# The check of w on GpSimd and its flag on ScalarE, in a fused attention and two-layer kernel

## Chip, core and metric

The kernel runs on one core of one Trainium2 chip. The metric is the device time of one execution in microseconds; smaller is better. The program before took 919.12 us, the median of three runs (918.99 to 919.40).

## What is computed

The reference is a linear attention with a decaying state, followed by two feed-forward layers, all in float32:

```python
for t in range(S):                       # S = 768, B = 4, H = 8, D = 48
    cur = einsum('bhd,bhe->bhde', u * k[t], v[t])
    y[t] = einsum('bhd,bhde->bhe', r[t], state + cur)
    state = w * state + einsum('bhd,bhe->bhde', k[t], v[t])
x = y.transpose(0, 2, 1, 3).reshape(B * S, H * D)      # 3072 x 384
x = ((x @ w_a) * (x @ w_b)) @ w_out                    # d_ff 1536
h = x @ w_in;  g = h * clip(h + 3, 0, 6) / 6
out = g @ w_out2                                       # d_ff 2048
```

w holds one decay for each of the 8 x 48 places, drawn between 0.85 and 0.95.

## The kernel before

The attention is computed by chunks of 128 steps: 6 chunks of the sequence times 4 batches are 24 chunks. Within a chunk r and k are scaled by powers of w and by their inverses, so that the decay becomes a product of matrices; masks take the part above the diagonal away, and the weight of a step on itself, from u, is put on the diagonal. Such powers only stay in range when w does. So the program first looks whether all of w lies in 0.75 to 1.33 (`W_MIN`, `W_MAX`). It makes a flag, every engine reads the flag (`decide`) and branches: to the chunked form, or to a general path that steps through the sequence. With these inputs the chunked form is taken.

The feed-forward layers split each float32 operand into a high and a low part and add three products. TensorE does the first four chunks ahead of layer 1; the 20 others are woven into layer 1 at fixed slots, then layer 2 follows. The engines run their own instruction streams, written out by hand, and meet at semaphores.

The change lies in the first microseconds, before the branch. There the order is this:

- **SyncE** (`first_loads`) issues the load of w and u (`w_u_col`), then `first_rk` for four chunks and `first_v` for two, then reads the flag and goes on with the weights (`w_raw`).
- **GpSimd** fills `three` and builds the masks (`make_masks`: one memset and eight selects, L487), clears the state (L1270), and reads the flag.
- **VectorE** (`guard_and_tables`) clears `zeros` (L1192) and sets the ones of the power table (L1193). It waits for w, compares it with both bounds (L1196 and L1198, results in `in_range`), scans the powers of w (L1201, four scans), takes TensorE's count, compares it (L1204) and turns it into an integer flag (L1206). Then come two reciprocals (L1208, L1209), the product r times k of the first chunk (L1049, waits for the first `first_rk`), the second table (L591), and its own reading of the flag. In `vector_fast` follow the scaling of r and k (L1044) and the masks (L1067, L1072).
- **ScalarE** makes a first activation, so that its table is loaded (L1279), and reads the flag. Then it copies the scale of the keys (L994), later the own weights of the first chunk (L1002), and from them eight diagonals (L854).
- **TensorE** multiplies zeros, to be kept busy (`keep_warm`, L756; the number is that of 128 columns), counts what is in range by four matmuls of one column (L1293), multiplies zeros again, then computes the own weights of the first chunk (L630) and its weights (L614) in `first_chunks`.

The tests for the count are a sum of 3.0 over 112 partitions x 4 columns: 1344 when all is in range.

Of the kernel before, what the change touches and what calls it, by code (L numbers as in the profile page):

```python
# [20 lines left out]
ALU = mybir.AluOpType  # L21
ACT = mybir.ActivationFunctionType
AX = mybir.AxisListType

P = 128
# [13 lines left out]
W_MIN, W_MAX = 0.75, 1.33  # L39
# [8 lines left out]
def build(nc, r, k, v, w, u, w_a, w_b, w_out, w_in2, w_out2, rk_turned, natural, w_u_pairs, outT):  # L48
# [11 lines left out]
    NP = H // 2  # L60
# [18 lines left out]
    with ExitStack() as ctx:  # L79
# [27 lines left out]
        with ExitStack() as setup:  # L107

            in_range = sb("in_range", [P, NP], of=setup)
            all_in = sb("all_in", [1, 1], of=setup)  # L110
            inv_fine = sb("inv_fine", [P, NP, FINE + 1], of=setup)
            inv_coarse = sb("inv_coarse", [P, NP, COARSE + 1], of=setup)
            zeros = sb("zeros", [P, CH], of=setup)
            tab_sT = sb("tab_sT", [P, NP, CH], of=setup)
# [192 lines left out]

        count_ps = acc_ps[0:1, 1, 0:1]
        HD = H * D
# [166 lines left out]


        def make_masks(pool):

# [16 lines left out]
            keep_where(P, every, 1, -1, MID, 1, ALU.is_equal)  # L496
            keep_where(P + MID, every, 1, -1, 0, 1, ALU.is_equal)
            keep_where(2 * P, low_half, 1, -1, 0, 1, ALU.is_gt)
            keep_where(late, every, 1, -1, MID, NP // 2, ALU.is_gt)
# [683 lines left out]

        def guard_and_tables(dve):

            links = [0]

            def link(ins):
# [6 lines left out]
            dve.wait_ge(s_w_u, 16)  # L1195
            dve.tensor_scalar(in_range[0:W2], w_col[0:W2], W_MIN, None, ALU.is_ge).then_inc(s_guard, 1)  # L1196
            dve.wait_ge(s_guard, 1)
            dve.scalar_tensor_tensor(out=in_range[0:W2], in0=w_col[0:W2], scalar=W_MAX, in1=in_range[0:W2],  # L1198
                                     op0=ALU.is_le, op1=ALU.mult).then_inc(s_guard, 1)
            for p in range(NP):  # L1200
                link(dve.tensor_tensor_scan(power[0:W2, p, 1:CH + 1], w_col[0:W2, p:p + 1].to_broadcast([W2, CH]),  # L1201
                                            zeros[0:W2, :], 1.0, ALU.mult, ALU.add))
            dve.wait_ge(s_count, 1)
            dve.tensor_scalar(all_in[:], count_ps, 3.0 * W2 * NP - 1.0, None, ALU.is_ge).then_inc(s_guard, 1)  # L1204
            dve.wait_ge(s_guard, 3)
            dve.tensor_copy(flag[:], all_in[:]).then_inc(s_flag, 1)  # L1206
            dve.wait_ge(s_set, links[0])
# [47 lines left out]
        with nc.Block() as block:  # L1255
# [10 lines left out]
            @block.gpsimd  # L1266
            def _(pool):
                nc.gpsimd.memset(three[:], 3.0).then_inc(s_three, 1)
                make_masks(pool)
                nc.gpsimd.memset(state[:], 0.0).then_inc(s_zero, 1)  # L1270
                flag_pool = decide(pool)
                with pool.If(flag_pool == 1):
                    pool_fast(pool)
                with pool.Else():
                    pool_general(pool)
            @block.scalar
            def _(act):
                act.wait_ge(s_three, 1)
                nc.scalar.activation(first_use[:], three[:], ACT.Copy)  # L1279
                flag_act = decide(act)  # L1280
                with act.If(flag_act == 1):
                    scalar_fast(act)
                with act.Else():
                    scalar_general(act)
                evacuate_last(act)
            @block.tensor
            def _(pe):
                pe.wait_ge(s_set, 1)
                keep_warm(pe, 4)
                pe.wait_ge(s_three, 1)  # L1290
                pe.wait_ge(s_guard, 2)
                for p in range(NP):
                    mm = pe.matmul(count_ps, in_range[0:W2, p:p + 1], three[0:W2, :], start=(p == 0), stop=(p == NP - 1))  # L1293
                mm.then_inc(s_count, 1)
                keep_warm(pe, 4)
                keep_warm(pe, 2)
                first_chunks(pe)
# [3 lines left out]
            def _(dve):  # L1301
                guard_and_tables(dve)
                flag_dve = decide(dve)
# [176 lines left out]
```

## Time and profile before

| | |
|---|---|
| median of three runs | 919.12 us (918.99 to 919.40) |
| the profiled execution's own time | 919.12 us |
| its span, first to last instruction | 917.3 us |
| TensorE busy | 911.9 us (99%) |
| VectorE busy | 369.5 us (40%) |
| ScalarE busy | 329.5 us (36%) |
| GpSimd busy | 184.3 us (20%) |

The profile is of one execution. The own time is longer than the span by what lies before the first and behind the last instruction. PE is TensorE, PEld its weight loads, DVE VectorE, ACT ScalarE, POOL GpSimd, and SPq the queue of SyncE that issues DMAs. A duration of a timeline row that merges several instructions (x4) reaches from the start of the first to the end of the last. The chain is followed back from the last instruction, at each step to what released it.

### The profile page before, as it was taken

The numbers are of one execution on the slowest core, as the hardware profiler recorded it, in microseconds if no ns is written. First come the engines' busy times: TensorE is split into PE (matmuls) and PEld (weight loads), VectorE is DVE, ScalarE is ACT, GpSimd is POOL, SyncE is SP. The second block draws the span as 40 slices with busy tenths as digits, with TensorE's granted clock in tenths as the row PEclk, the third lists the DMA queues.
The fourth block names the chain that finished last, engine by engine and source line by source line (L and its number), as shares of the span: only waits on it lengthen the run. The fifth ranks groups of instructions, "written<-read, shape, count | busy, mean of one in ns | idle before, by whom it ended". The sixth has DMA issues, their size and how long they took to land.

```text
span 917.3 us, 15108 instructions
## 1 busy us (share of the span) xinstructions
PE 911.9 (99%) x6400; PEld 746.4 (81%) x6400; DVE 369.5 (40%) x607; ACT 329.5 (36%) x651; POOL 184.3 (20%) x168
## 2 busy tenths in 40 slices
PE   8999999999999999999999999999999999999998
PEld 6788888888888888888888888888888888888887
DVE  7746344525443343334222343343343343343332
ACT  6645323232333233242221343433333333333333
POOL 5976102111111111010755570000000000000000
PEclk9999999999999999999999999999999999999999
DMA  8653211121120121131311210100200100100000
GB/s 307 198 167 108 90 50 62 55 90 56 56 110 34 56 110 55 38 129 48 115 50 55 78 50 1 65 5 1 69 1 0 70 1 7 64 0 1 35 1 36
DMA packets 24281, 57.84 MB, mean 63 GB/s; under 512 B 2320, under 2 KB 8080, under 8 KB 24208
## 3 DMA queue, kind: packets, MB, share of 16 engines
q1 hardware_dynamic: 19808, 48.18, 15.6%
q10 hardware_dynamic: 4400, 8.65, 2.5%
q8 instruction: 50, 0.82, 0.4%
q14 instruction: 23, 0.19, 0.1%
HBM read 47.39 MB, written 9.44 MB: 62 GB/s over the span
## 4 chain that ended last, share of the span: by engine, by line
PE 98%; DVE 1%; DMA 0%; ACT 0%; issue 0%; SPq 0%; DVEq 0%; ACTq 0%
PE up_ps L722 32%; PE up_ps L799 21%; PE acc_ps L736 16%; PE acc_ps L813 11%; PE att_ps L813 11%; PE att_ps L614 2%; PE att_ps L677 1%; PE att_ps L682 1%; PE att_ps L646 1%; PE att_ps L663 1%; PE att_ps L671 1%; DMA first_rk<-in_rk_turned 0%; ACT A L854 0%; DVE first_rk L1044 0%; DVE first_A L1067 0%
## 5 line engine op out<-in xcount | busy, mean ns | idle before, releaser
L722 PE MATMUL up_ps<-x_cut,w_up 128*128 128x512 f32 x1296 | 307.3, 391 | 0.2 <-ACT x_cut L867 0.2
L722 PEld LDWEIGHTS up_ps<-x_cut,w_up 128*128 128x128 f32 x1296 | 241.7, 188 | 52.9 <-issue 3.0
L926 ACT ACTIVATE g_cut<-tmp 128x512 fp32r<-128x512 f32 x168 | 106.2, 632 | 214.4 <-DVE tmp L1149 141.6
L1157 DVE SCALAR_TENSOR_TENSOR g_cut<-tmp,g_cut 128x512 fp32r<-128x512 f32 x168 | 125.2, 745 | 117.5 <-ACT g_cut L926 117.5
L736 PE MATMUL acc_ps<-g_cut,w_down 128*128 128x512 f32 x648 | 157.3, 390 | 0.0
L736 PEld LDWEIGHTS acc_ps<-g_cut,w_down 128*128 128x128 f32 x648 | 121.3, 188 | 26.0 <-issue 0.6
L1151 DVE SCALAR_TENSOR_TENSOR tmp<-tmp,up_ps 128x512 f32<-128x512 f32 x96 | 66.1, 689 | 182.9 <-ACT tmp L920 182.9
L920 ACT ACTIVATE tmp<-up_ps,three 128x512 f32<-128x512 f32 x96 | 66.2, 690 | 171.0 <-PE up_ps L799 171.0
L1149 DVE TENSOR_TENSOR tmp<-tmp,up_ps 128x512 f32<-128x512 f32 x72 | 49.5, 688 | 169.7 <-PE up_ps L722 169.6
L799 PE MATMUL up_ps<-x_cut,w_up 128*128 128x512 f32 x432 | 105.7, 389 | 0.0
L799 PE MATMUL up_ps<-x_cut,w_in_first 128*128 128x512 f32 x432 | 105.4, 389 | 0.0
L799 PEld LDWEIGHTS up_ps<-x_cut,w_up 128*128 128x128 f32 x432 | 81.1, 188 | 16.8
L799 PEld LDWEIGHTS up_ps<-x_cut,w_in_first 128*128 128x128 f32 x432 | 81.1, 188 | 16.8
L918 ACT ACTIVATE tmp<-up_ps 128x512 f32<-128x512 f32 x72 | 43.0, 598 | 112.4 <-PE up_ps L722 112.4
L513 POOL TENSOR_TENSOR nat<-nat 128x384 f32<-128x384 f32 x20 | 23.6, 1180 | 278.9 <-DMA nat<-in_natural 278.9
L813 PE MATMUL att_ps<-g_cut,w_up 128*128 128x512 f32 x324 | 79.3, 389 | 0.0
L813 PE MATMUL acc_ps<-g_cut,w_up 128*128 128x512 f32 x324 | 79.3, 389 | 0.0
L813 PEld LDWEIGHTS att_ps<-g_cut,w_up 128*128 128x128 f32 x324 | 60.8, 188 | 12.6
L813 PEld LDWEIGHTS acc_ps<-g_cut,w_up 128*128 128x128 f32 x324 | 60.8, 188 | 12.6
L854 ACT ACTIVATE A<-masks_sb,own 128x128 f32<-128x128 f32 x160 | 50.3, 388 | 5.6 <-DVE own L1060 5.6
L243 POOL TENSOR_TENSOR w_up<-w_raw,w_up 128x512 fp32r<-128x512 f32 (+2 forms) x42 | 47.3, 1140 | 6.9 <-ACT w_up L237 5.2
L1101 DVE TENSOR_TENSOR x_cut<-att_ps,x_cut 128x384 fp32r<-128x384 f32 x21 | 11.7, 557 | 60.3 <-ACT x_cut L867 60.3
(109 smaller groups left out, 557.2 us busy)
## 6 DMA issues: line engine op xcount, KB each, us to landing
nat<-in_natural SPq DMA_DIRECT2D x20, 704.0 KB, 6.0
rkT<-in_rk_turned SPq DMA_DIRECT2D x20, 512.0 KB, 3.6
w_raw<-in_moe_w_out SPq DMA_DIRECT2D x28, 192.0 KB, 2.4
layer_out_T<-stage ACTq DMA_DIRECT2D x6, 768.0 KB, 3.4
x_cut<-layer_out_T SPq DMA_DIRECT2D x6, 768.0 KB, 4.3
outT<-stage ACTq DMA_DIRECT2D x5, 768.0 KB, 3.3
w_raw<-in_moe_w_in SPq DMA_DIRECT2D x12, 256.0 KB, 4.6
first_rk<-in_rk_turned SPq DMA_DIRECT2D x4, 512.0 KB, 5.6
```

Source lines behind the costliest of these rows:

```text
L243: nc.gpsimd.tensor_tensor(out=pieces[m][1](LO), in0=raw_of(m), in1=pieces[m][1](HI).bitcast(F32), op=ALU.subtract).then_inc(s_w_cut, 1)
L722: mm = pe.matmul(up_ps[:, m, :], w_up[i // PB][:, a, m, c, cols], x_cut[:, t % 2, b, c, :], start=(z == 0), stop=(z == len(order) - 1))
L736: mm = pe.matmul(acc_ps[:, j, :], w_down[:, a, i, j * P:(j + 1) * P], g_cut[:, (t * N1 + i) % GR, b, :], start=(i == 0 and z == 0), stop=( ...
L799: mm = pe.matmul(up_ps[:, i % 2, :], in2_at(a, c, i), x_cut[:, t % 2, b, c, :], start=(c == 0 and z == 0), stop=(c == KC - 1 and z == 2))
L813: mm = pe.matmul(sums(t)[:, j, :], wo2_at(a, i)[:, j * P:(j + 1) * P], g_cut[:, n % GR, b, :], start=(i == 0 and z == 0), stop=(last and z ...
L854: ins = nc.scalar.activation(A_at(q, half)[:, p, :], id_sb[p // 2], ACT.Copy, scale=mine[:, h:h + 1])
L918: nc.scalar.activation(tmp[:, i % 2, :], src, ACT.Copy).then_inc(s_act1, 1)
L920: nc.scalar.activation(tmp[:, i % 2, :], src, ACT.Relu, bias=three[:, 0:1]).then_inc(s_act1, 1)
L926: nc.scalar.activation(g_cut[:, n % GR, HI, :], tmp[:, n % 2, :], ACT.Copy, scale=1.0 if n < TILES * N1 else 1.0 / 6.0).then_inc(s_gh, 1)
L1149: dve.tensor_tensor(out=tm, in0=tm, in1=up_ps[:, 1, :], op=ALU.mult).then_inc(s_g, 1)
L1151: dve.scalar_tensor_tensor(out=tm, in0=tm, scalar=6.0, in1=up_ps[:, n % 2, :], op0=ALU.min, op1=ALU.mult).then_inc(s_g, 1)
L1157: dve.scalar_tensor_tensor(out=lo, in0=tmp[:, n % 2, :], scalar=1.0 if n < TILES * N1 else 1.0 / 6.0, in1=hi.bitcast(F32), op0=ALU.mult, o ...
```

## The change

Both comparisons of w go from VectorE to GpSimd (`find_in_range`): two comparisons into two tiles and a product of the two, between the fourth and the fifth select of `make_masks`. The flag is now made by ScalarE, in one activation that reads TensorE's count in PSUM: Relu(count + 1 - 1344) is 1 when all is in range and 0 otherwise, and is written as an integer. The bias stands in a tile of one value, `all_but_one`, that GpSimd fills first. TensorE's wait for the comparisons goes from the second to the third step of their semaphore, the count lies in another bank of PSUM (`att_ps` in place of `acc_ps`), and the last of the two warming matmuls behind the count has 128 columns instead of 256. `guard_and_tables` becomes `tables_of_powers`. The order of SyncE's loads stays.

```diff
--- before.py
+++ after.py
@@ -107,7 +107,8 @@
         with ExitStack() as setup:
 
             in_range = sb("in_range", [P, NP], of=setup)
-            all_in = sb("all_in", [1, 1], of=setup)
+            not_above = sb("not_above", [P, NP], of=setup)
+            all_but_one = sb("all_but_one", [1, 1], of=setup)
             inv_fine = sb("inv_fine", [P, NP, FINE + 1], of=setup)
             inv_coarse = sb("inv_coarse", [P, NP, COARSE + 1], of=setup)
             zeros = sb("zeros", [P, CH], of=setup)
@@ -305,7 +306,7 @@
         def x_view(tile, z, q):
             return x_cut[:, tile % 2, z, :, cols_of(q)]
 
-        count_ps = acc_ps[0:1, 1, 0:1]
+        count_ps = att_ps[0:1, 0, 0:1]
         HD = H * D
         by_head = lambda x: x.rearrange("s (h d) -> s h d", h=H)
         A_of = lambda q: first_A[:, q % 2] if 2 <= q < B else A[:, q % 2]
@@ -475,6 +476,15 @@
                 sp.dma_start(outT_v[:, j, cols], st[:, j, :]).then_inc(s_st, 16)
 
 
+        def find_in_range(pool):
+
+            pool.wait_ge(s_w_u, 16)
+            nc.gpsimd.tensor_scalar(in_range[0:W2], w_col[0:W2], W_MIN, None, ALU.is_ge).then_inc(s_guard, 1)
+            nc.gpsimd.tensor_scalar(not_above[0:W2], w_col[0:W2], W_MAX, None, ALU.is_le).then_inc(s_guard, 1)
+            pool.wait_ge(s_guard, 2)
+            nc.gpsimd.tensor_tensor(out=in_range[0:W2], in0=in_range[0:W2], in1=not_above[0:W2],
+                                    op=ALU.mult).then_inc(s_guard, 1)
+
         def make_masks(pool):
 
 
@@ -495,6 +505,7 @@
             keep_where(MID, every, 1, -1, MID, 1, ALU.is_equal)
             keep_where(P, every, 1, -1, MID, 1, ALU.is_equal)
             keep_where(P + MID, every, 1, -1, 0, 1, ALU.is_equal)
+            find_in_range(pool)
             keep_where(2 * P, low_half, 1, -1, 0, 1, ALU.is_gt)
             keep_where(late, every, 1, -1, MID, NP // 2, ALU.is_gt)
             keep_where(late + NP // 2 * MID, low_half, 1, -1, 0, NP // 2, ALU.is_gt)
@@ -1181,7 +1192,7 @@
                     if i == 4 and t + 1 < TILES:
                         x2_low(dve, t + 1)
 
-        def guard_and_tables(dve):
+        def tables_of_powers(dve):
 
             links = [0]
 
@@ -1193,17 +1204,9 @@
             link(dve.memset(power[:, :, 0:1], 1.0))
             dve.wait_ge(s_set, links[0])
             dve.wait_ge(s_w_u, 16)
-            dve.tensor_scalar(in_range[0:W2], w_col[0:W2], W_MIN, None, ALU.is_ge).then_inc(s_guard, 1)
-            dve.wait_ge(s_guard, 1)
-            dve.scalar_tensor_tensor(out=in_range[0:W2], in0=w_col[0:W2], scalar=W_MAX, in1=in_range[0:W2],
-                                     op0=ALU.is_le, op1=ALU.mult).then_inc(s_guard, 1)
             for p in range(NP):
                 link(dve.tensor_tensor_scan(power[0:W2, p, 1:CH + 1], w_col[0:W2, p:p + 1].to_broadcast([W2, CH]),
                                             zeros[0:W2, :], 1.0, ALU.mult, ALU.add))
-            dve.wait_ge(s_count, 1)
-            dve.tensor_scalar(all_in[:], count_ps, 3.0 * W2 * NP - 1.0, None, ALU.is_ge).then_inc(s_guard, 1)
-            dve.wait_ge(s_guard, 3)
-            dve.tensor_copy(flag[:], all_in[:]).then_inc(s_flag, 1)
             dve.wait_ge(s_set, links[0])
             link(dve.reciprocal(inv_fine[0:W2], fine[0:W2]))
             link(dve.reciprocal(inv_coarse[0:W2], coarse[0:W2]))
@@ -1266,6 +1269,7 @@
             @block.gpsimd
             def _(pool):
                 nc.gpsimd.memset(three[:], 3.0).then_inc(s_three, 1)
+                nc.gpsimd.memset(all_but_one[:], 1.0 - 3.0 * W2 * NP).then_inc(s_three, 1)
                 make_masks(pool)
                 nc.gpsimd.memset(state[:], 0.0).then_inc(s_zero, 1)
                 flag_pool = decide(pool)
@@ -1275,8 +1279,11 @@
                     pool_general(pool)
             @block.scalar
             def _(act):
-                act.wait_ge(s_three, 1)
+                act.wait_ge(s_three, 2)
                 nc.scalar.activation(first_use[:], three[:], ACT.Copy)
+
+                act.wait_ge(s_count, 1)
+                nc.scalar.activation(flag[:], count_ps, ACT.Relu, bias=all_but_one[:, 0:1]).then_inc(s_flag, 1)
                 flag_act = decide(act)
                 with act.If(flag_act == 1):
                     scalar_fast(act)
@@ -1288,18 +1295,18 @@
                 pe.wait_ge(s_set, 1)
                 keep_warm(pe, 4)
                 pe.wait_ge(s_three, 1)
-                pe.wait_ge(s_guard, 2)
+                pe.wait_ge(s_guard, 3)
                 for p in range(NP):
                     mm = pe.matmul(count_ps, in_range[0:W2, p:p + 1], three[0:W2, :], start=(p == 0), stop=(p == NP - 1))
                 mm.then_inc(s_count, 1)
                 keep_warm(pe, 4)
-                keep_warm(pe, 2)
+                keep_warm(pe, 1)
                 first_chunks(pe)
                 tensor_layer1(pe)
                 tensor_layer2(pe)
             @block.vector
             def _(dve):
-                guard_and_tables(dve)
+                tables_of_powers(dve)
                 flag_dve = decide(dve)
                 with dve.If(flag_dve == 1):
                     vector_fast(dve)
```

VectorE, from the memset of the power table to the reciprocals. Names in brackets are the semaphores waited for: `w_and_u_loaded` is the load of w and u, `in_range_counted` TensorE's count. Before:

```order
L1193 MEMSET tab_rk 128x4
L1196 TENSOR_SCALAR in_range<-w_u_col 112x4 [waits w_and_u_loaded,table_chain]
L1198 SCALAR_TENSOR_TENSOR in_range<-w_u_col,in_range 112x4 [waits guard_chain]
L1201 SCALAR_TENSOR_TENSOR tab_rk<-w_u_col,zeros 112x128 x4
L1204 TENSOR_SCALAR all_in<-acc_ps 1x1 [waits in_range_counted]
L1206 CAST flag<-all_in 1x1 [waits guard_chain]
L1208 RECIPROCAL inv_fine<-tab_rk 112x68 [waits table_chain]
L1209 RECIPROCAL inv_coarse<-tab_rk 112x36
L1049 TENSOR_TENSOR prod<-first_rk 112x512 [waits first_rk_loaded0]
```

The same place in the changed program:

```order
L1204 MEMSET tab_rk 128x4
L1208 SCALAR_TENSOR_TENSOR tab_rk<-w_u_col,zeros 112x128 [waits w_and_u_loaded,table_chain]
L1208 SCALAR_TENSOR_TENSOR tab_rk<-w_u_col,zeros 112x128 x3
L1211 RECIPROCAL inv_fine<-tab_rk 112x68 [waits table_chain]
L1212 RECIPROCAL inv_coarse<-tab_rk 112x36
L1060 TENSOR_TENSOR prod<-first_rk 112x512 [waits first_rk_loaded0]
```

Four instructions are gone, and with them the wait for TensorE's count; the scans wait for the load of w themselves.

GpSimd, from its first memset to the memset of the state, before:

```order
L1268 MEMSET three 128x1
L492 MEMSET masks_sb 128x576
L487 ISA
L487 AFFINE_SELECT masks_sb<-masks_sb 128x64 [waits ones_set]
L487 AFFINE_SELECT masks_sb<-masks_sb 128x64 x3
L487 AFFINE_SELECT masks_sb<-masks_sb 64x64
L487 AFFINE_SELECT masks_sb<-masks_sb 128x128
L487 AFFINE_SELECT masks_sb<-masks_sb 64x128
L487 AFFINE_SELECT masks_sb<-masks_sb 64x64 [waits masks_made]
L1270 MEMSET state_fast 128x1024 [waits masks_made]
```

And in the changed program, from the second memset to the last select:

```order
L1272 MEMSET all_but_one 1x1
L502 MEMSET masks_sb 128x576
L497 ISA
L497 AFFINE_SELECT masks_sb<-masks_sb 128x64 [waits ones_set]
L497 AFFINE_SELECT masks_sb<-masks_sb 128x64 x3
L482 TENSOR_SCALAR in_range<-w_u_col 112x4 [waits w_and_u_loaded]
L483 TENSOR_SCALAR not_above<-w_u_col 112x4
L485 TENSOR_TENSOR in_range<-in_range,not_above 112x4 [waits guard_chain]
L497 AFFINE_SELECT masks_sb<-masks_sb 64x64
L497 AFFINE_SELECT masks_sb<-masks_sb 128x128
L497 AFFINE_SELECT masks_sb<-masks_sb 64x128
L497 AFFINE_SELECT masks_sb<-masks_sb 64x64 [waits masks_made]
```

One memset and three instructions on w have come in, the latter with a wait for the load in front of the last four selects.

ScalarE, from its start to the first work behind the branch, in the changed program (before, the row with `flag<-att_ps,all_but_one` is missing, and nothing else differs):

```order
L1283 ACT_TABLE_LOAD
L1283 ACTIVATE first_use<-three 128x1 [waits three_set]
L1286 ACTIVATE flag<-att_ps,all_but_one 1x1 [waits in_range_counted]
L1256 TENSOR_LOAD flag [waits flag_ready]
L1256 ISA x2
L1288 COMPARE_AND_BRANCH
L1005 ACTIVATE tab_sT<-tab_rk 112x256 [waits table_chain]
```

The new row waits for TensorE's count, and ScalarE's own reading of the flag stands behind it.

## Rows read from the trace of the kernel before

**Rows 1.** The page: span, and busy time of each engine.

```profile
span 917.3 us, 15108 instructions
...
PE 911.9 (99%) x6400; PEld 746.4 (81%) x6400; DVE 369.5 (40%) x607; ACT 329.5 (36%) x651; POOL 184.3 (20%) x168
```

**Rows 2.** The page: shares of the chain that ended last.

```profile
PE 98%; DVE 1%; DMA 0%; ACT 0%; issue 0%; SPq 0%; DVEq 0%; ACTq 0%
```

**Rows 3.** The chain in order of time: start us, duration us, what.

```profile
1.25 3.95 DMA first_rk<-in_rk_turned
...
5.23 0.70 DVE prod L1049
...
5.97 1.06 PE acc_ps L630 x12
...
7.13 0.18 ACT own_first L1002
...
7.34 2.45 ACT A L854 x8
...
9.91 0.74 DVE A L1067
...
20.55 2.37 PE up_ps L722 x9
```

**Rows 4.** Timeline of VectorE, 0 to 8 us: start, us, engine, line, what.

```profile
2.60 0.17 DVE L1196 TENSOR_SCALAR in_range<-w_u_col 112x4 f32<-112x4 f32 x1 [1.52 <-DMA w_u_col<-in_w_u_pairs]
2.80 0.17 DVE L1198 SCALAR_TENSOR_TENSOR in_range<-w_u_col,in_range 112x4 f32<-112x4 f32 x1
2.89 1.36 DVE L1201 TENSOR_TENSOR_SCAN tab_rk<-w_u_col,zeros 112x128 f32<-112x128 f32 x4
4.17 0.12 DVE L1204 TENSOR_SCALAR all_in<-acc_ps 1x1 f32<-1x1 f32 x1
4.33 0.14 DVE L1206 CAST flag<-all_in 1x1 int32<-1x1 f32 x1
4.40 0.56 DVE L1208 RECIPROCAL inv_fine<-tab_rk 112x68 f32<-112x68 f32 x1
4.88 0.31 DVE L1209 RECIPROCAL inv_coarse<-tab_rk 112x36 f32<-112x36 f32 x1
```

**Rows 5.** Timeline of GpSimd, before and at the scans: same columns.

```profile
0.80 0.10 POOL L1268 MEMSET three<- 128x1 f32 x1 [0.29 <-POOLq L1433]
...
1.48 0.24 POOL L487 TENSOR_SCALAR_AFFINE_SELECT masks_sb<-masks_sb 128x64 f32<-128x64 f32 x1
...
3.02 0.32 POOL L487 TENSOR_SCALAR_AFFINE_SELECT masks_sb<-masks_sb 64x64 f32<-64x64 f32 x1
...
3.40 0.95 POOL L1270 MEMSET state_fast<- 128x1024 f32 x1
```

**Rows 6.** TensorE's timeline; then one stretch, granted clock third number from the end.

```profile
3.12 0.34 PE L1293 MATMUL acc_ps<-three,in_range 112*1 112x1 f32 x8
...
3.39 2.02 PE L756 MATMUL up_ps<-zeros 128*128 128x512 f32 x2
...
4.41 1.22 PE L756 MATMUL up_ps<-zeros 128*128 128x512 f32 x2
...
5.25 0.59 PE L756 MATMUL up_ps<-zeros 128*128 128x256 f32 x2
...
6.95 1.12 PE L756 MATMUL up_ps<-zeros 128*128 128x512 f32 x2
...
1.00:2.00 1.00, 0.88 (x1) 0.50 (x2) 0.08 (x2) 1.00 (x1) 0.93 (x4) 1.00 0.05 3
```

**Rows 7.** Timeline of SyncE's queue and of ScalarE.

```profile
3.14 1.18 SPq L366 DMA_DIRECT2D first_v<-in_natural  x2
...
5.34 0.82 ACT L994 ACTIVATE tab_sT<-tab_rk 112x256 f32<-112x256 f32 x3 [3.04 <-DVE inv_coarse L1209]
5.40 0.94 SPq L232 DMA_DIRECT2D w_raw<-in_moe_w_a  x2
```

## The prediction

> **What bounds the kernel now.** The page comes first, for the span and the engines' busy time. The span is 917.3 us and TensorE is busy in 911.9 of it [rows 1], so only 5.4 us of its time are not matmuls. The shares of the chain that ended last say the same: 98% is PE, and DVE has 1% [rows 2]. A change to four VectorE instructions of 0.1 to 0.2 us can therefore only tell where TensorE isn't yet the bound, which is the start. For that I read the chain in order of time, and its first pieces are the argument [rows 3]. It begins with the load of the first `first_rk`, which lands at 1.25 + 3.95 = 5.20 us. Behind it come VectorE's product (5.23), TensorE's own products (5.97), ScalarE's copy and eight diagonals (7.13 to 9.79) and VectorE's first mask (9.91). About ten more microseconds of such hand-overs lead to 20.55 us, where layer 1 begins on TensorE, and from there the chain is TensorE nearly throughout. The change edits only what lies between 0.8 and 5.9 us. So the question is whether the product at 5.23 or the matmuls at 5.97 can start at another time.
>
> The product sits on a near tie. VectorE's timeline [rows 4] has the second reciprocal at 4.88 for 0.31 us, so VectorE is free at 5.19; the load lands at 5.20. VectorE is as late as the load, but no later.
>
> **The change on VectorE.** It loses the two comparisons (L1196 and L1198) and the two instructions of the flag (L1204 and L1206). The scans now start when w lands, at 2.60 where the first comparison stood, instead of at 2.89 [rows 4]: 0.29 us earlier, so they end at 2.60 + 1.36 = 3.96. The reciprocals follow their last result directly. They started at 4.40 behind the flag; from the first start to the end of the second they take 5.19 - 4.40 = 0.79, so they now end at about 3.98 + 0.79 = 4.77. VectorE is ready for the product 0.42 us earlier. The product still waits for the load at 5.20, and SyncE's queue ahead of that load is unchanged (w and u first, then the four `first_rk`). The gain on the path is 5.19 to 5.20, so **nothing**; the 0.42 us become a wait for DMA. This is where the gain stops. The bounds are 0 and 0.42 us, and I take 0.
>
> **On GpSimd.** A memset of one value is added; the one in front of it, `three`, took 0.10 [rows 5], so at most 0.10. Then three instructions on 112x4 stand between the fourth select and the fifth. The trace has no such instruction on this engine. Its nearest rows are a memset of one column per partition, 0.10, and selects on 128x64 and 64x64, 0.24 and 0.32 [rows 5]. I take 0.20 each, near the select, since it too reads and writes, with fewer elements here. Four selects from 1.58 on, of 0.24 at most, are done by 2.54, so the wait for w (2.60) is what starts the three. The first two overlap to 0.3 in all, the third waits for both and takes 0.20, and with 0.05 for the hand-over that is 2.60 + 0.55 = 3.15; by the upper bound, 3 x 0.32 = 0.96, it is 3.56. The four later selects, the memset of the state and GpSimd's reading of the flag move back by 0.5 to 1.0 us. Before, the selects ended at 3.34 and the state's memset at 4.35 [rows 5], and their first readers are ScalarE at 7.13 [rows 3] and later, so a microsecond is covered twice over.
>
> The Trainium skill, GPSIMD Engine Reference, section Engine selection, speaks against this move: two-input elementwise work is about twice as slow there as on VectorE. With twice the 0.17 us of L1196 for each of the three, an estimate by that page, the end is 2.60 + 1.02 = 3.62, within 0.1 of my upper bound, and the sum stays the same.
>
> **On TensorE.** The count (four matmuls of one column, 0.34 us) started at 3.12, when the first warming matmul let it [rows 6]. It now waits for GpSimd: 3.20, or 3.65 by the upper bound; call the lateness d, 0.1 to 0.5 us. Behind it stand the warming matmuls, first 512 columns, then 256, which the change cuts to 128. What follows them matters: the own products at 5.97, which waited for VectorE's product, not for TensorE, free at 5.25 + 0.59 = 5.84. From the starts [rows 6]: one pass of 512 columns took 4.41 - 3.39 = 1.02 us, the next 5.25 - 4.41 = 0.84, and at 6.95 two took 1.12, or 0.56 each. The granted clock reads 1.00 already in the stretch from 1 to 2 us, which is the upper level, 2.4 GHz, and TensorE works there 0.88 of the time. But the passes nearly halve, so I read that the array really rose from the lower level, 1.2 GHz, after it had been busy from about 1.1 us on, and with 0.84 between 1.02 and 0.56, at 4.41 + 0.61 x 1.02 = 5.03. After the change with d = 0.1: the second pass starts at 4.51, does 0.51 of itself until 5.03 and the rest by 5.30; two passes of 128 columns at a quarter of 0.56 end at 5.58. With d = 0.5 the end is 5.80. TensorE meets 5.97 as long as d is below about 0.75, that is, GpSimd done by 3.85. Cost: nothing; the cover is TensorE's idle time before 5.97.
>
> **On ScalarE and SyncE.** The flag is made by one activation of 1x1 from PSUM: 0.18 us by the copy of 128x8 from PSUM [rows 3], 0.10 after the count ends, as between the end of the own products at 5.97 + 1.06 = 7.03 and 7.13. So the flag is ready at 3.20 + 0.34 + 0.10 + 0.18 = 3.82 (4.3 by the upper bound) instead of 4.33 + 0.14 = 4.47. ScalarE sat idle for the 3.04 us before 5.34 [rows 7], so nothing is queued behind its new wait except its own reading of the flag. SyncE can't use all of this: its issue of `first_v` runs from 3.14 to 4.32 [rows 7], and before it waited only from there to the flag at 4.47. Its first w_raw issue moves from 5.40 to about 5.25, and the issues behind it too. These transfers queue behind those that the chain needs, on the same queue, and no piece of the chain before 20.55 waits for one; worth 0. VectorE reads the flag after it has dispatched the product and the table, as before.
>
> **Sum.** Product 0, own products 0, flag 0: 0.0 us on the profiled execution. Its own time is 919.12 us, equal to the median of the three runs (919.12), so I predict 919.1. A measurement of this kernel can tell about 0.2% (1.8 us) from no change, and all the time on the path between 2.60 and 5.97 is 3.4 us.
>
> **Rivals.** *GpSimd is held by VectorE's scans, and TensorE is late.* Both now start when w lands, both read it, and the scans run back to back until 3.96. If GpSimd's instructions wait for all four, they end at 3.96 + 0.60 = 4.56 and the count at 4.60 + 0.34 = 4.94; that is d = 1.5, past the deciding 0.75. With the clock risen at 5.03 as before, 2.5 passes end at 5.03 + (2.5 - 0.09) x 0.56 = 6.38: 0.4 us late, 919.5. If the idle 1.4 us put off the rise of the clock as well, they end at 4.94 + 2.5 x 1.02 = 7.49 (+1.5), and the own products, 1.06 long, may double (+1.1). Then ScalarE's copy and diagonals, and with them the mask at 9.91, come 2.6 us late: 921.7, slower. Against it speaks the last select: it ran from 3.02 to 3.34 [rows 5], wholly beside the scans that began at 2.89 [rows 4], and took 0.32 where it should have been held to the end of a scan first. For it: 0.32 is more than 0.24. I give the mild form 0.07 and the hard one 0.05.
>
> The Trainium skill, SBUF — State Buffer, section Who interferes with whom, has this as a rule: a VectorE instruction with two SBUF inputs holds off a GpSimd instruction that reads SBUF, for its whole length. By that rule the mild form or worse should come; the trace's select of 0.32 agrees at most in part.
>
> *The load is not the last to arrive.* In the profiled execution load and VectorE are 0.01 us apart. If in most executions the load lands earlier than 5.20, the chain gains what VectorE gave up, up to 0.42 us: 918.7. For it speaks the tie alone, which would be a coincidence; against it, that the trace names the load and that the times of three runs lie within 0.4 us. Chance 0.13.
>
> *The change doesn't do what it says:* an activation with Relu could bring a second table load in front of the flag. The built program has one load on ScalarE in both kernels, and ScalarE's 3 us of idle time would take much of another. It changes no time and I fold it into the forecast.
>
> **How the numbers follow.** Forecast (within 0.3 us of 919.1) 0.71; a gain by the early load, 0.13, 918.7; GpSimd held with the clock in time, 0.07, 919.5; with the clock late, 0.05, 921.7; anything else, 0.04, half of it faster by over 0.2% and half within. The slower case is 2.6 us, over the 1.8 us; all other listed ones are below it. So faster 0.02, same 0.71 + 0.13 + 0.07 + 0.02 = 0.93, slower 0.05. The range reaches from the early load, less 0.2 for the spread of the runs, 918.5, to the mild form of the first rival, plus 0.3 for the same, 919.8. It leaves out the hard form.
>
> **What would show it.** In the profile after: VectorE's scans start at 2.6 and its reciprocals end near 4.8, followed by a new wait of about 0.4 us for `first_rk`; GpSimd's three instructions end between 3.1 and 3.6; the count starts just behind; flag at 3.8 to 4.3; product at 5.2, own products near 5.97, first mask at 9.9, layer 1 at 20.5. I'm wrong if the own products start after 6.1 (TensorE late), if the second warming pass no longer shortens (clock), or if the product starts clearly before 5.2 (the load was not the bound).

## The result and the profile after

| | before | changed |
|---|---|---|
| median | 919.50 us, 22 runs | 924.02 us, 22 runs |
| lowest to highest | 918.94 to 920.11 | 918.88 to 925.07 |
| profiled execution | 919.12, span 917.3 | 924.59, span 922.9 |

The ratio is 1.0034, with a 95% interval of 1.0023 to 1.0045: slower, and outside the forecast range of 918.5 to 919.8. It follows the means, here and below; the medians alone give 1.0049. In the runs below, three executions far outside all others, which no run explains, are left out of counts, medians and ratios: one of 3280 us with the kernel before, one of 1534 in e2 and one of 1533 in e8. The median tells less than the single times. Of the 22 executions 6 took 918.9 to 919.9 us, as before; 4 took 920.9 to 921.8; 12 took 924.0 to 925.1. The kernel before has its 22 within 1.2 us. The change has made the time fall into three groups.

The page of the changed kernel, whose profiled execution is of the slowest group:

```profile
span 922.9 us, 15107 instructions
...
PE 917.5 (99%) x6400; PEld 751.6 (81%) x6400; DVE 368.8 (40%) x603; ACT 329.4 (36%) x652; POOL 185.3 (20%) x172
...
PE 99%; ACT 0%; DMA 0%; DVE 0%; issue 0%; POOL 0%; DVEq 0%
```

Against [rows 1] TensorE is busy for 5.6 us more with as many matmuls, and against [rows 2] VectorE's 1% has left the chain. The chain in order of time says where (start, duration, what):

```profile
0.80 1.59 DMA w_u_col<-in_w_u_pairs
...
3.09 0.21 POOL in_range L485
3.30 0.14 issue
3.44 0.34 PE att_ps L1300 x8
3.77 2.43 PE up_ps L767 x4
6.21 1.37 PE acc_ps L641 x12
7.58 2.01 PE up_ps L767 x2
9.58 1.49 PE up_ps L625 x32
11.07 1.67 PE acc_ps L641 x12
...
20.97 0.18 ACT own_first L1013
...
25.93 2.34 PE up_ps L733 x9
```

Layer 1 begins at 25.93 instead of 20.55 [rows 3], 5.38 of the span's 5.6 us. The other 0.2 is not placed. From 3.44 to 20.94 the chain is TensorE without a break, where before it was a relay of four engines.

The timelines of VectorE, GpSimd and ScalarE, each in its first microseconds:

```profile
2.49 1.43 DVE L1208 TENSOR_TENSOR_SCAN tab_rk<-w_u_col,zeros 112x128 f32<-112x128 f32 x4 [1.41 <-DMA w_u_col<-in_w_u_pairs]
3.96 0.58 DVE L1211 RECIPROCAL inv_fine<-tab_rk 112x68 f32<-112x68 f32 x1
4.45 0.32 DVE L1212 RECIPROCAL inv_coarse<-tab_rk 112x36 f32<-112x36 f32 x1
5.03 0.69 DVE L1060 TENSOR_TENSOR prod<-first_rk 112x512 f32<-112x512 f32 x1 [0.26 <-DMA first_rk<-in_rk_turned]
```

```profile
2.46 0.24 POOL L482 TENSOR_SCALAR in_range<-w_u_col 112x4 f32<-112x4 f32 x1
2.78 0.22 POOL L483 TENSOR_SCALAR not_above<-w_u_col 112x4 f32<-112x4 f32 x1
3.09 0.20 POOL L485 TENSOR_TENSOR in_range<-in_range,not_above 112x4 f32<-112x4 f32 x1
```

```profile
3.81 0.25 ACT L1286 ACTIVATE flag<-att_ps,all_but_one 1x1 int32<-1x1 f32 x1 [1.52 <-PE att_ps L1300]
```

These came nearly as forecast. VectorE is free at 4.77 (forecast 4.77), waits 0.26 us for the load, and the product starts 0.20 us earlier than before, since here the load landed at 5.0. GpSimd ends at 3.29 (forecast 3.15 to 3.56), the flag at 4.06 (3.8 to 4.3). What is different is TensorE's timeline:

```profile
1.12 2.07 PE L767 MATMUL up_ps<-zeros 128*128 128x512 f32 x2 [1.12 <-DVE tab_rk L1204]
3.44 0.34 PE L1300 MATMUL att_ps<-three,in_range 112*1 112x1 f32 x8 [0.24 <-POOL in_range L485]
3.70 2.50 PE L767 MATMUL up_ps<-zeros 128*128 128x512 f32 x4
6.00 1.58 PE L641 MATMUL acc_ps<-w_u_col,prod 112*128 112x64 f32 x12
7.51 2.08 PE L767 MATMUL up_ps<-zeros 128*128 128x512 f32 x2
...
15.18 1.58 PE L641 MATMUL acc_ps<-w_u_col,prod 112*128 112x64 f32 x12
...
18.55 1.40 PE L625 MATMUL up_ps<-first_rk 48*64 48x128 f32 x32
19.89 1.04 PE L641 MATMUL acc_ps<-w_u_col,prod 112*128 112x64 f32 x12
```

The own products of the first chunk start at 6.00, as before (5.97), but the warming pair of 512 columns behind them takes 2.08 us where it took 1.12 [rows 6]. The next own products take up to 1.7 us until 16.8 and 1.04 only at 19.89. Only TensorE is slower: ScalarE's copy `own_first` takes 0.18 us and VectorE's product 0.69 in both kernels. I read from these durations that TensorE ran at the lower of its two levels, 1.2 GHz, until about 19.7 us, within the row at 18.55; before, it rose to 2.4 GHz ahead of 5.97. The granted clock does not show it. The table of stretches gives it as the third number from the end, and in this stretch, with slow passes throughout, it reads 1.00, the upper level:

```profile
8.00:9.00 1.00, 1.00 (x2) 0.01 (x1) 0.90 (x2) 1.00 (x4) 0.00 (x0) 1.00 1.00 384
```

### The profile page after: what moved, and what is told of

It reads as the page before. It is cut to its first block, busy times and chain, and to the rows that moved or that the text cites. A ratio compares the mean times of both kernels' runs of the same rounds, so it can differ in the third digit from the quotient of the medians.

```text
span 922.9 us, 15107 instructions
## 1 busy us (share of the span) xinstructions
PE 917.5 (99%) x6400; PEld 751.6 (81%) x6400; DVE 368.8 (40%) x603; ACT 329.4 (36%) x652; POOL 185.3 (20%) x172
## 4 chain that ended last, share of the span: by engine, by line
PE 99%; ACT 0%; DMA 0%; DVE 0%; issue 0%; POOL 0%; DVEq 0%
PE up_ps L733 32%; PE up_ps L810 21%; PE acc_ps L747 16%; PE acc_ps L824 11%; PE att_ps L824 11%; PE att_ps L625 2%; PE att_ps L688 1%; PE att_ps L693 1%; PE att_ps L657 1%; PE att_ps L674 1%; PE acc_ps L641 1%; PE att_ps L682 1%; PE up_ps L767 0%; PE up_ps L625 0%; PE acc_ps L688 0%; DMA w_u_col<-in_w_u_pairs 0%
## 5 line engine op out<-in xcount | busy, mean ns | idle before, releaser
L810 PEld LDWEIGHTS up_ps<-x_cut,w_in_first 128*128 128x128 f32 x432 | 81.1, 188 | 16.8
L810 PEld LDWEIGHTS up_ps<-x_cut,w_up 128*128 128x128 f32 x432 | 81.1, 188 | 16.8
```

What stands on the lines that cost most here:

```text
L810: mm = pe.matmul(up_ps[:, i % 2, :], in2_at(a, c, i), x_cut[:, t % 2, b, c, :], start=(c == 0 and z == 0), stop=(c == KC - 1 and z == 2))
```

## The experiments

The question is which part of the change puts off the rise of the clock. Three things changed ahead of 6 us on TensorE: it waits 0.24 us for GpSimd ahead of the count (the gap), it does 128 warming columns less, and the count comes at 3.44 instead of 3.12. Below, 512 | 512, 256 means the warming columns ahead of the count and behind it. Executions are sorted by time into "early" (under 920.4 us), "middle" (to 923.6) and "late" (up to 925.7); the names are those of the rise of the clock, which the profiles place at 5.3 to 8, at about 11, and at about 20 us. The gap is that of the one profiled execution.

| kernel | warming | gap in the profile | early | middle | late | median |
|---|---|---|---|---|---|---|
| before, 125 executions | 512 \| 512, 256 | none | 123 | 2 | 0 | 919.3 to 919.8 |
| changed | 512 \| 512, 128 | 0.24 | 6 | 4 | 12 | 924.02 |
| e1 | 512 \| 512, 256 | 0.28 | 4 | 3 | 5 | 922.61 |
| e2 (of before) | 512 \| 512, 128 | 0.13 | 2 | 5 | 3 | 921.74 |
| e3 | 512, 128 \| 512 | none | 5 | 4 | 3 | 921.04 |
| e4 | 512 \| 512, 512 | 0.49 | 1 | 6 | 4 | 921.07 |
| e5 | 512 \| 512, 256 | none | 11 | 0 | 0 | 919.61 |
| e6 | 512 \| 512, 256 | 0.28 | 5 | 2 | 3 | 920.84 |
| e7 | 512, 128 \| 512, 128 | none | 8 | 2 | 1 | 920.00 |
| e8 | 512, 256 \| 384 | none | 6 | 1 | 4 | 919.47 |
| e9 (of before) | 512 \| 512, 256 | 0.29 | 5 | 2 | 5 | 922.09 |
| e10 and e11 | 512, 256 \| 512 | none | 20 | 2 | 0 | 919.12, 919.17 |

The cuts of the code below are shown against the changed kernel for e1, e3, e4, e7, e8, e10 and e11, and against the kernel before for e2, e5, e6 and e9; `...` stands for lines left out.

### e1: the 256 columns restored

```diff
                 keep_warm(pe, 4)
-                keep_warm(pe, 1)
+                keep_warm(pe, 2)
```

> The changed kernel, with the second warming matmul behind the count at 256 columns, as before, instead of 128. In the changed kernel's profile TensorE's passes of 512 columns still take 1.04 us at 7.51 (0.56 before), and everything on it up to about 19 us is slow: that is the loss. Theory A (the gap): what puts off the rise is that TensorE waits for GpSimd from 3.19 to 3.44 us. The gap is untouched here, so the times stay spread between 919 and 925 with a median over 922. Theory B (the shorter warming): what puts it off is the 128 columns taken away. Then the times fall back to 919.0 to 920.0, median 919.4, or less by the 0.2 us by which the load landed earlier.

Measured: 922.61 us, 919.79 to 924.99; ratio 1.0033, 1.0020 to 1.0046. As theory A expected. A third is early: with the gap the rise is uncertain even with all columns. Its profiled execution (924.83):

```profile
3.47 0.34 PE L1300 MATMUL att_ps<-three,in_range 112*1 112x1 f32 x8 [0.28 <-POOL in_range L485]
3.74 2.93 PE L767 MATMUL up_ps<-zeros 128*128 128x512 f32 x4
...
5.61 1.06 PE L767 MATMUL up_ps<-zeros 128*128 128x256 f32 x2
...
6.46 1.58 PE L641 MATMUL acc_ps<-w_u_col,prod 112*128 112x64 f32 x12
7.97 2.08 PE L767 MATMUL up_ps<-zeros 128*128 128x512 f32 x2
```

The same four passes took 2.45 us before (3.39 to 5.84) and take 2.93 here, and the own products start 0.5 us later for it. (The row at 5.61 is the last two of the four, from a narrower stretch of the timeline.)

### e2: the shorter warming alone

```diff
                 keep_warm(pe, 4)
-                keep_warm(pe, 2)
+                keep_warm(pe, 1)
```

> The kernel before, with that warming matmul cut to 128 columns and nothing else: no gap before the count, which starts at 3.12. Theory A: 919.0 to 920.1 as before, and passes of 0.56 us at 6.95. Theory B: spread from 919 to 925, median over 921.

Measured: 921.74 us (921.93 with the execution of 1534 us), ratio 1.0030, 1.0017 to 1.0043. This is theory B's outcome, where e1 was A's. Neither alone is right: each part by itself puts off the rise. (In the profiled execution w landed late enough for a gap of 0.13 us as well.) The profiled execution (922.12) is of the middle group and shows what sets it apart, a rise at about 11 us:

```profile
6.04 1.74 PE L630 MATMUL acc_ps<-w_u_col,prod 112*128 112x64 f32 x12
...
9.72 1.56 PE L614 MATMUL up_ps<-first_rk 48*64 48x128 f32 x32
11.21 1.04 PE L630 MATMUL acc_ps<-w_u_col,prod 112*128 112x64 f32 x12
```

### e3: the 128 columns ahead of the count

```diff
                 keep_warm(pe, 4)
+                keep_warm(pe, 1)
                 pe.wait_ge(s_three, 1)
...
                 keep_warm(pe, 4)
-                keep_warm(pe, 1)
```

> The changed kernel, with the 128 columns moved from behind the count to ahead of it, so that TensorE still works while GpSimd compares; behind the count stand 512 columns alone. The sum of columns is the changed kernel's. Theory A: the gap of 0.25 us closes to under 0.1 and the times go back to 919.0 to 920.0. Theory B (too few columns): as the changed kernel, 919 to 925, median over 922; or worse, since TensorE then idles before its own products at about 5.8.

Measured: 921.04 us, 918.74 to 924.72; ratio 1.0019, 1.0004 to 1.0034. Neither theory's numbers: 5 of 12 are early, against 6 of 22 for the changed kernel, too few to call it better. With the gap closed the lack of columns is left.

### e4: 512 columns in the last warming matmul

```diff
-                keep_warm(pe, 1)
+                keep_warm(pe, 4)
```

> The changed kernel, with the second warming matmul at 512 columns instead of 128. TensorE is then busy until about 7.4 us by slow passes, or 6.5 if the clock rises in them, and the own products (ready at 5.7) start later than 6.0. Theory A: the rise still depends on the gap, so the spread stays and each time is up to 1.5 us longer, median over 923. Theory B: the rise always comes, and the cost is what the own products wait: 919.5 to 920.5, median near 920.

Measured: 921.07 us, 920.36 to 925.70; ratio 1.0030, 1.0016 to 1.0044. Neither theory fits. Seven of 11 lie at 920.4 to 921.1 and four at 925.4 to 925.7. I take the seven for early rises that pay for the own products' lateness; the one profile is of a late execution (925.53), so that isn't shown. More columns behind the gap may help (7 of 11 against 6 of 22), and don't make up for it. In the profile w came later too, and the gap was 0.49.

### e5: the flag on ScalarE alone

```diff
-            dve.wait_ge(s_count, 1)
-            dve.tensor_scalar(all_in[:], count_ps, 3.0 * W2 * NP - 1.0, None, ALU.is_ge).then_inc(s_guard, 1)
-            dve.wait_ge(s_guard, 3)
-            dve.tensor_copy(flag[:], all_in[:]).then_inc(s_flag, 1)
...
+                act.wait_ge(s_count, 1)
+                nc.scalar.activation(flag[:], count_ps, ACT.Relu, bias=all_but_one[:, 0:1]).then_inc(s_flag, 1)
```

> One part of the change alone: VectorE compares as before, ScalarE makes the flag, the warming matmuls as before (512 | count | 512, 256). The count starts near 3.1 us again, with no gap ahead of it. Theory A2 (the rise of the clock comes early only when TensorE is busy almost without a break from 1.1 to 6 us; a gap of 0.25 us ahead of the count or 0.3 us more behind the last warming pass each spoil it): no break, so 919.0 to 920.1, median 919.4. Rival D (what spoils it is the flag's new place, through the transfers and reads behind it that come earlier): spread from 919 to 925, median over 921.

Measured: 919.61 us, 919.03 to 919.92; ratio 1.0003, 0.9994 to 1.0012. All 11 early, as theory A2 expected. Nothing that the flag's new place costs or brings is clear of the noise. The profile:

```profile
3.17 0.34 PE L1303 MATMUL att_ps<-three,in_range 112*1 112x1 f32 x8
3.44 2.93 PE L766 MATMUL up_ps<-zeros 128*128 128x512 f32 x4
6.16 1.12 PE L640 MATMUL acc_ps<-w_u_col,prod 112*128 112x64 f32 x12
7.21 1.12 PE L766 MATMUL up_ps<-zeros 128*128 128x512 f32 x2
```

Here the clock rose at about 6.3, behind the warming passes instead of within them, and the own products are already near 1.04. They start 0.2 us later, and the execution took 919.57. So a rise a microsecond later than before still counts as early.

### e6: the comparisons on GpSimd alone

```diff
-            dve.tensor_scalar(in_range[0:W2], w_col[0:W2], W_MIN, None, ALU.is_ge).then_inc(s_guard, 1)
...
+            find_in_range(pool)
...
-                pe.wait_ge(s_guard, 2)
+                pe.wait_ge(s_guard, 3)
```

> The other part alone: GpSimd compares, VectorE makes the flag as before, the warming matmuls as before. The gap of 0.25 us ahead of the count is there. Theory A2: spread like the changed kernel with 256 columns restored (919.8 to 925, median 922.6). Rival D: 919.0 to 920.1.

Measured: 920.84 us, 919.25 to 925.40; ratio 1.0027, 1.0011 to 1.0043. The spread is there, five of ten executions above 920.4. So the loss comes with the comparisons, not with the flag. The profiled execution (919.91) is an early one, with the gap of 0.28 that stood before a late rise in e1:

```profile
6.46 1.35 PE L642 MATMUL acc_ps<-w_u_col,prod 112*128 112x64 f32 x12
7.75 1.13 PE L768 MATMUL up_ps<-zeros 128*128 128x512 f32 x2
```

The clock rose at about 7.3, within the own products. The size of the gap alone doesn't decide when.

### e7 and e8: warming that covers the wait for GpSimd

```diff
                 keep_warm(pe, 4)
+                keep_warm(pe, 1)
                 pe.wait_ge(s_three, 1)
```

> The changed kernel with 128 columns more, ahead of the count: 512, 128 | count | 512, 128. The sum of columns is that of the kernel before and of the run with 256 restored, which had a median of 922.6; only the gap ahead of the count is filled. Theory A2: the early rise comes nearly always, and the own products start at about 6.2, so 919.2 to 920.2, median near 919.6. Rival E (it is the late count, or the sum of columns, not the gap): median over 921.5.

Measured: 920.00 us, 918.89 to 925.05; ratio 1.0009, 0.9997 to 1.0020. The median lies between the two expectations, and 8 of 11 are early: more than with the gap (4 of 12 in e1), though on so few executions that may be chance. The profiled execution (921.36) is of the middle group:

```profile
1.12 2.50 PE L767 MATMUL up_ps<-zeros 128*128 128x512 f32 x4 [1.12 <-DVE tab_rk L1204]
3.55 0.34 PE L1301 MATMUL att_ps<-three,in_range 112*1 112x1 f32 x8
3.82 2.50 PE L767 MATMUL up_ps<-zeros 128*128 128x512 f32 x4
...
11.12 1.10 PE L641 MATMUL acc_ps<-w_u_col,prod 112*128 112x64 f32 x12
```

TensorE has no break from 1.12 on, and yet the clock rose only at about 11.2.

Then e8:

```diff
                 keep_warm(pe, 4)
+                keep_warm(pe, 2)
                 pe.wait_ge(s_three, 1)
...
-                keep_warm(pe, 4)
-                keep_warm(pe, 1)
+                keep_warm(pe, 3)
```

> The changed kernel with 512, 256 | count | 384: no break at all from 1.1 us to the count at about 4.0, and the last pass ends near 5.9, so the own products start at about 5.9. Theory A2: always the early rise, 918.8 to 919.8, median 919.1 to 919.4: the same as before or 0.2 us less, since VectorE no longer comes as late as the load. Rival E: spread, median over 921.

Measured: 919.47 us (920.20 with the execution of 1533 us); ratio 1.0023, 1.0006 to 1.0040. Six of 11 early, four above 924. Theory A2, in its simple form (busy without a break is enough), is wrong: e7's profile shows a rise at 11.2 with no break before it, and e8's profile has none from 1.12 to 5.8, though it is of an early execution (919.47). With 384 columns behind the count, e8 also has the changed kernel's sum of columns, 1152.

### e9: a gap in the kernel before

```diff
                 pe.wait_ge(s_guard, 2)
+                pe.wait_ge(s_masks, MASK_PARTS)
```

> The kernel before, with one more wait ahead of TensorE's count: for all eight selects of GpSimd, which end at 3.35 to 3.4 us. Nothing is moved, VectorE compares and makes the flag, the warming matmuls are 512 | count | 512, 256. The count starts at about 3.45 instead of 3.12 and TensorE idles about 0.25 us in front of it. VectorE reads the count at 4.17 at the earliest in any case, so the flag keeps its time. Theory A2 (the gap itself): about half of the executions between 920.5 and 925, median 919.5 to 922.5, most above 920. Rival F (something else of GpSimd's comparisons, not TensorE's gap): 918.9 to 920.1 in all.

Measured: 922.09 us, 919.64 to 925.06; ratio 1.0034, 1.0020 to 1.0048: the changed kernel's ratio, from one added wait. The profiled execution (920.30):

```profile
3.49 0.34 PE L1294 MATMUL acc_ps<-three,in_range 112*1 112x1 f32 x8 [0.29 <-POOL masks_sb L487]
3.76 2.93 PE L756 MATMUL up_ps<-zeros 128*128 128x512 f32 x4
6.48 1.57 PE L630 MATMUL acc_ps<-w_u_col,prod 112*128 112x64 f32 x12
7.98 1.12 PE L756 MATMUL up_ps<-zeros 128*128 128x512 f32 x2
```

VectorE wrote the flag at 4.33 for 0.14 us as before. The clock rose just ahead of 7.98, and this execution is early. Nothing is moved between engines here, so GpSimd's comparisons themselves are not to blame; what counts is that TensorE stands still for 0.3 us and counts later.

### e10 and e11: no gap, and all the columns

```diff
                 keep_warm(pe, 4)
+                keep_warm(pe, 2)
                 pe.wait_ge(s_three, 1)
...
                 keep_warm(pe, 4)
-                keep_warm(pe, 1)
```

> The changed kernel with 512, 256 | count | 512: no gap ahead of the count, and 128 columns more than in the run with 512, 256 | count | 384, of which 5 of 12 executions lay above 924. Theory A3 (both must hold: no gap, and full passes until about 6 us): the rise comes early in nearly all executions, 919.1 to 920.1, median 919.5, with the own products starting at 6.2 to 6.4. Rival G (the count's own late place, 4.0 instead of 3.1 us, is what makes the rise uncertain): a third or more above 920.8.

Measured: 919.12 us, 918.79 to 919.68, all 11 early; ratio 0.9996, 0.9988 to 1.0005. The profile (919.35):

```profile
3.98 0.34 PE L1301 MATMUL att_ps<-three,in_range 112*1 112x1 f32 x8
4.25 1.76 PE L767 MATMUL up_ps<-zeros 128*128 128x512 f32 x2
5.84 0.97 PE L641 MATMUL acc_ps<-w_u_col,prod 112*128 112x64 f32 x12
6.74 1.12 PE L767 MATMUL up_ps<-zeros 128*128 128x512 f32 x2
```

Two passes of 512 in 1.76, between 2.07 and 1.12: the clock rose inside the second. The result is theory A3's, and against rival G: the count starts at 3.98 here and all are early. (The five of 12 in the expectation include the execution of 1533 us.) Layer 1 began at 20.37, 0.18 before that of [rows 3].

> The same kernel as the last one (512, 256 | count | 512), once more, to see whether it holds: if its 919.12 was luck in a spread of the kind seen with 384 columns behind the count (5 of 12 above 924), some of these executions lie above 920.8. If both conditions are met by it, all lie between 918.7 and 919.8, and the median is 0.1 to 0.3 us below that of the kernel before.

Measured: 919.17 us, 918.87 to 923.41; ratio 0.9999, 0.9989 to 1.0010. Nine early, two not (921.24 and 923.41), so the 11 of 11 of e10 may have been in part luck. It is nearly cured, 20 of 22, against 6 of 22 for the changed kernel and 6 of 11 for e8, which differs by 128 columns alone. The medians lie 0.2 and 0.6 us below those of the kernel before in the same batches, and both intervals take in 1: as fast as before, not shown to be faster. No kernel tried beats the one before.

### All kernels put together

| | no gap over 0.13 us | gap of 0.24 to 0.29 us |
|---|---|---|
| 1280 warming columns | 162 of 169 early (before, e5, e7, e10, e11) | 14 of 34 (e1, e6, e9) |
| 1152 warming columns | 13 of 33 (e2, e3, e8) | 6 of 22 (changed) |

Either edit alone takes the certainty of the early rise away, and about as much of it. That both together do more than one isn't shown by so few executions. Nor are the fields of the table all of one kind: e7, at 8 of 11, lies below the others of its field (154 of 158). e4, with 1536 columns and a gap of 0.49, stands outside the table.

## Why the prediction was wrong

**VectorE, right.** The four instructions went, the reciprocals ended at 4.77, and what was won became a wait of 0.26 us for the load. **ScalarE, SyncE, right.** The flag came at 4.06 and the first `w_raw` issue at 5.31 (forecast 5.25); e5, the flag alone, measured 1.0003.

**GpSimd, right in size.** The three instructions took 0.24, 0.22 and 0.20 us, by my 0.20. But they start 0.3 us apart, the second included, so they end 0.83 after the first start where I had added 0.55. Nor was the two-input one, 0.20, twice VectorE's 0.17. The work behind them moved by more than my 0.5 to 1.0: the state's memset ended at 5.57 instead of 4.35, still ahead of the 7.13 that I had named for the first readers. The rival that VectorE's scans hold GpSimd off didn't come: the first comparison ran from 2.46 to 2.70 and the scans from 2.49, the third ended at 3.29 and not behind the scans at 3.92, and the scans took 1.43 against 1.36 before, so if anything was held it was for 0.07 us. The rule of the Trainium skill (SBUF — State Buffer, section Who interferes with whom), by which a VectorE instruction with two SBUF inputs contends with a GpSimd instruction that reads SBUF, is not borne out by these rows.

**TensorE, wrong; the step that failed** is "TensorE meets 5.97 as long as d is below about 0.75 ... Cost: nothing". TensorE did meet it: with d = 0.32 the own products started at 6.00. That was luck in part: their product was ready at 5.72, and with d = 0.32 my sum has TensorE free at about 5.7; it was the warming passes, slow to their end, that held them until 6.00. I had priced only when TensorE is free, and taken the moment of the clock's rise, 5.03, as given. Two faults lie in that.

- The reading was wrong. I took the shortening from 1.02 to 0.84 us between two passes of 512 columns as a sign of the rise. In the changed kernel, all slow, the same passes start at 3.70, 4.72 and the next at 5.57, 1.02 and 0.85 apart:

```profile
4.72 1.27 PE L767 MATMUL up_ps<-zeros 128*128 128x512 f32 x2
...
5.57 0.64 PE L767 MATMUL up_ps<-zeros 128*128 128x128 f32 x2
```

  (Both rows are from narrower stretches of the timeline.) What does differ is the sum of the four passes behind the count, 2.45 us before against 2.93 in e1, e5 and e9, and within it the two passes of 256 columns, 0.59 us [rows 6] against 1.06 in e1. The rise before came at about 5.3, where these two begin.
- The rise is not given. It depends on what TensorE did before, and a gap of 0.3 us (e9), or 128 columns of 1280 less (e2), is enough to take more than half of the executions out of the early group (7 of 12, and 8 of 10), where the kernel before loses 2 of 125. I named the mechanism ("if the idle 1.4 us put off the rise of the clock as well"), but tied it to a long idle time and to the scans, with a chance of 0.05 and a price of 2.6 us. A rise put off to 7 or 8 us costs little (e6 and e9, 919.91 and 920.30 us). The middle and the late group lie some 2 and 5 us up, because there it comes at about 11 (10.9 to 11.2 in e2, e3 and e7) or about 20 us (19.7 to 20.2 in the changed kernel, e1 and e4).

What the changed kernel lost thus comes from two edits on TensorE, each enough alone, and the change's own subject, the place of the comparisons, is the cause of only one. The 128 columns, which I had counted as time won, hurt by themselves.

None of my three signs of being wrong caught it. The own products started before 6.1; the second warming pass seemed to shorten, as it does at the lower level too; and the product did start before 5.2, at 5.03, but only because the load landed earlier in this execution, and VectorE still waited for it.

The Trainium skill, TensorE: Matmul & The Clock Gate, section What's actually happening, says that the chip sets this clock by how busy TensorE has lately been, that the observation runs free of the kernel's start, and that the same kernel therefore meets the change at different points from run to run. The groups at 919, 921.5 and 924.5 us in one and the same kernel agree with it, though the kernel before met the rise early in 123 of 125. I had not used that page; it would have spoken for a rival in which less work ahead of the rise puts it off.

**Open.** That the clock is what slows TensorE is read from durations, which grow by half to nine tenths for every form of matmul; the granted clock reads 1.00 throughout. Which of the two edits weighs more is not settled; the groups are of 10 to 22 executions. Each kernel has one profile, so what sorts the executions of one kernel into groups isn't seen: w lands at another time in each (GpSimd's first comparison starts at 2.46 to 2.76 in the profiles), but e1 and e6, with w at the same time and the same gap, went two ways. e8 has 128 columns fewer than e10; why e7, with as many as e10 and no gap, still failed in 3 of 11 is open, though at 8 of 11 against 20 of 22 the two may not differ at all. The late count by itself, at 3.98, did not spoil e10 and e11; with a gap ahead of it the two were not separated. So what exactly the chip asks for before it raises the clock is left open; the runs show only what upsets it.

## What to carry to other kernels

Work that keeps TensorE busy at the start is not slack: before cutting it or putting a wait in its midst, ask what it does to the moment when the clock rises, and price the whole slow start (here 5 us), not the idle 0.3 us. Judge such a change by the spread of many executions; one profile shows one group. And put a wait for another engine behind enough warming work that it has ended by then, as in e10, and keep the warming work behind it whole.

## What the hardware showed that was not expected

- The time of one kernel falls into three groups, and in the 13 profiles the clock rises at 5.3 to 8, about 11 or about 20 us. The last costs 5.4 us at the start of layer 1 (25.93 against 20.55).
- TensorE can work without a break and stay slow: from 1.12 to about 11.2 us in e7, and from 3.44 to about 19.7 in the changed kernel.
- One added wait of 0.29 us (e9) raised the median by 2.8 us.
- The granted clock of the profile reads 1.00 in the stretches of all these starts, slow or not. Only the durations of like matmuls tell: 2.08 against 1.12 us for two passes of 512 columns, 1.58 to 1.74 against 1.04 us for twelve own products.
- GpSimd takes 0.20 to 0.24 us for an instruction on 112x4, with starts 0.3 us apart; VectorE took 0.17 for either comparison in the kernel before.
